# A fused attention, token-mixing and channel-mixing kernel: second tile's loads behind the first tile's heads, global-key terms on GpSimd, and three changes of order

## The reference, cut to what matters

```python
B, H, S, D = 2, 8, 768, 64                                # d_model = 512
scores = q @ k^T / 8 - slope_h * dist(is_global, is_local); masked by keep
a = exp(scores - max) / (sum + 1e-9);  x = a @ v          # [2, 768, 512]

h  = relu(x^T @ w_tok1) @ w_tok2                          # over tokens, 768 -> 256 -> 768
u  = x + h^T
x2 = u + relu(u @ w_ch1) @ w_ch2                          # 512 -> 1536 -> 512

theta = x2 @ w_theta                                      # 512 x 512
z_r, z_i = x2 * cos(theta), x2 * sin(theta)
y  = w_tok_r @ z_r + w_tok_i @ z_i                        # 768 x 768, over tokens
u2 = x2 + y
out = u2 + relu(u2 @ w_ch)                                # 512 x 512
```

## Time and profile before

| what | value |
|---|---|
| median of 3 timed runs | 496.13 us (496.01 to 496.19) |
| profiled execution | 497.82 us, of which span 496.0 us and 1.8 us around it |
| TensorE busy | 487.6 us (98% of the span) |
| VectorE, ScalarE, GpSimd busy | 325.8, 192.3, 267.7 us |
| mean granted TensorE clock | 0.996 |
| chain that ended last | TensorE 87%, VectorE 11%, the rest 2% |

### The profile page before, as it was taken

One profiled execution on the slowest core, in us unless ns is written; L12 is line 12 of the kernel. 1 busy time (PEld: TensorE's weight loads), 2 busy tenths in 40 slices (PEclk: granted clock), 3 DMA queues, 4 the chain that ended last, 5 costly groups with the idle time before them and its releaser, 6 DMA issues.

```text
span 496.0 us, 8394 instructions
## 1 busy us (share of the span) xinstructions
PE 487.6 (98%) x2917; PEld 445.6 (90%) x2917; DVE 325.8 (66%) x797; ACT 192.3 (39%) x413; POOL 267.7 (54%) x315
## 2 busy tenths in 40 slices
PE   7999999999999999999999999999989999999997
PEld 5999999899999999889999998888878899888897
DVE  7998999569535433399625436798887665655552
ACT  6999898555112121146112214344232321321230
POOL 3575566599798983739798882554930310000040
PEclk9999999999999999999999999999989999999999
DMA  7897675522132232104242242133102211000002
GB/s 239 326 304 242 239 219 147 157 85 84 58 95 85 83 110 85 44 0 128 64 129 85 72 134 72 65 110 125 42 2 60 67 66 64 0 1 0 2 32 96
DMA packets 27083, 49.81 MB, mean 100 GB/s; under 512 B 3360, under 2 KB 17696, under 8 KB 27040
## 3 DMA queue, kind: packets, MB, share of 16 engines
q1 hardware_dynamic: 27040, 49.26, 31.6%
HBM read 39.81 MB, written 3.15 MB: 87 GB/s over the span
## 4 chain that ended last, share of the span: by engine, by line
PE 87%; DVE 11%; issue 1%; ACT 1%; DMA 1%; DVEq 0%
PE bank L323 63%; PE bank L1800 7%; PE bank L1506 5%; PE bank L1536 4%; PE bank L1539 4%; PE bank L1520 2%; PE bank L1518 2%; DVE act_raw L1224 2%; DVE zc L1240 1%; DVE zs L1258 1%; DVE act_raw L1218 1%; DVE za L1234 1%; DVE tile L1202 1%; DVE zb L1253 1%; DMA counts<-both_counts 1%
## 5 line engine op out<-in xcount | busy, mean ns | idle before, releaser
L323 PE MATMUL bank<-wsplit 128*128 128x256 f32 (+2 forms) x816 | 148.8, 338 | 0.0
L323 PEld LDWEIGHTS bank<-wsplit 128*128 128x128 f32 x816 | 134.1, 188 | 13.3
L710 POOL TENSOR_TENSOR wsplit<-wraw,wsplit 128x512 fp32r<-128x512 f32 (+1 forms) x77 | 102.1, 1327 | 41.4 <-ACT wsplit L883 25.5
L323 PE MATMUL bank<-wsplit,zs 128*128 128x512 f32 (+1 forms) x576 | 105.0, 342 | 2.1 <-DVE zs L1258 2.1
L323 PEld LDWEIGHTS bank<-wsplit,zs 128*128 128x128 f32 x576 | 90.9, 191 | 16.7 <-issue 2.5
L778 POOL TENSOR_TENSOR split<-act_raw,split 128x384 fp32r<-128x384 f32 x12 | 12.5, 1079 | 105.5 <-ACT split L1008 105.5
L652 POOL TENSOR_TENSOR wsplit<-qk_raw,wsplit 64x256 fp32r<-64x256 f32 x46 | 38.0, 827 | 33.1 <-DVE wsplit L1051 32.8
L323 PE MATMUL bank<-split,wsplit 128*128 128x384 f32 x276 | 53.8, 339 | 0.4 <-DVE zb L1235 0.3
L704 POOL CAST wsplit<-wraw 128x512 fp32r<-128x512 f32 (+1 forms) x59 | 36.1, 612 | 26.9 <-PE bank L323 17.5
L323 PEld LDWEIGHTS bank<-split,wsplit 128*128 128x128 f32 x276 | 47.3, 188 | 1.1 <-DVE zb L1235 0.5
L1371 DVE SCALAR_TENSOR_TENSOR wsplit<-bank,wsplit 128x384 fp32r<-128x384 f32 x30 | 16.7, 558 | 38.1 <-ACT wsplit L961 26.9
(11 more groups left out here) (126 smaller groups left out, 749.9 us busy)
## 6 DMA issues: line engine op xcount, KB each, us to landing
wraw<-weights SPq DMA_DIRECT2D x28, 512.0 KB, 3.4
qk_raw<-qk SPq DMA_DIRECT2D x23, 528.0 KB, 4.5
wraw<-weights SPq DMA_DIRECT2D x8, 768.0 KB, 4.1
vt<-v SPq DMA_DIRECT2D x10, 520.0 KB, 4.6
xT<-turned SPq DMA_DIRECT2D x64, 48.0 KB, 2.0
out<-act_raw SPq DMA_DIRECT2D x16, 192.0 KB, 1.9
xT<-turned_early SPq DMA_DIRECT2D x16, 96.0 KB, 2.7
xT<-wraw SPq DMA_DIRECT2D x32, 48.0 KB, 2.0
```

Of the source, the lines that this page charges most:

```text
L323: mm = pe.matmul(dst, lhs(a), rhs(c), start=first and i == 0, stop=last and i == 2, skip_group_check=True)
L710: ins = pool.tensor_tensor(dst[:, cols], src[:, cols], hi[:, cols].bitcast(F32), ALU.subtract)
```

## The change

- SyncE waits for heads 4 to 7 of the first tile before it issues the second tile's transfers (and all that stands behind them).
- GpSimd instead of VectorE makes the global keys' terms and the first tile's bias of them, seven instructions instead of six, ahead of its first `queries_lo`. VectorE's wait for `slopes_ready` is gone; it waits for `gbias_ready` before it builds the other tiles' part.
- `WARM` goes from 13 to 11, `CHAN_FROM` from 3 to 5.
- VectorE makes `z_to_lo(g, 0)` before `tile_to_lo` and not behind it.
- For the last i of the last batch, TensorE makes three blocks and not two between `angles(0)` and the first product; one fewer stands at the end.

```diff
-WARM = 13
+WARM = 11
-CHAN_FROM = 3
+CHAN_FROM = 5
...
             load_queries_keys(0)
+            sp.wait_ge(qk_in[0][1], 16)
             for n in range(UNITS):
...
+            def find_global_terms():
+                ng, nl = cf[:, 0:1], cf[:, 2:3]
+                pool.tensor_scalar(c_gkey, c_gkey, ng, None, ALU.is_lt)
+                link(pool.tensor_scalar(c_gkeep, c_grel, nl, None, ALU.is_ge))
+                link(pool.tensor_tensor(c_gkeep, c_gkeep, c_gkey, ALU.mult))
+                pool.tensor_scalar(c_gdrop, c_gkeep, -MASKED, MASKED, ALU.mult, ALU.add)
+                link(pool.tensor_scalar(c_gdist, c_gkeep, nl, -1.0 / SCALE, ALU.mult, ALU.mult))
+
+            def first_global_bias():
+                heads = c_gheads[:, 0:H * G].rearrange("p (h g) -> p h g", h=H)
+                link(pool.tensor_tensor(heads, ..., ALU.mult))
+                pool.tensor_tensor(gbias[:, :, 0, :], heads, ..., ALU.add).then_inc(gbias_ready, 1)
...
             pool.wait_ge(slopes_ready, H)
+            pool.wait_ge(consts, 4)
+            pool.wait_ge(counts_ready, 1)
+            find_global_terms()
+            first_global_bias()
             for m in range(FIRST, PAIRS):
                 queries_lo(m)
...
             keys_lo(0, 0)
-            find_global_terms()
-            dve.wait_ge(slopes_ready, H)
-            build_global_bias(0, 1)
...
                 if m == PAIRS - 1:
+                    dve.wait_ge(gbias_ready, 1)
                     build_global_bias(1, 2)
...
                         multiply_x(g)
+                    if g >= 2 and not (b and s == 0):
+                        z_to_lo(g, 0)
                     if g >= 2 and g + 2 < B * T:
                         tile_to_lo(B * T + g + 2)
-                    if g >= 2 and not (b and s == 0):
-                        z_to_lo(g, 0)
...
                         angles(0)
-                        block(i - 1, *blocks[0])
-                        block(i - 1, *blocks[1])
+                        for at in range(3):
+                            block(i - 1, *blocks[at])
                         pe.wait_ge(th_taken, 1)
...
-                        block(i - 1, *blocks[2 if ahead else 0])
+                        block(i - 1, *blocks[3 if ahead else 0])
...
-                        block(i - 1, *blocks[3 if ahead else 1])
+                        block(i - 1, *blocks[4 if ahead else 1])
...
-                    block(i - 1, *blocks[4 if ahead else 2])
+                    block(i - 1, *blocks[5 if ahead else 2])
...
-                    block(i - 1, *blocks[5])
+                    block(i - 1, *blocks[6 if ahead else 5])
...
-                    block(i - 1, *blocks[6])
+                    if not ahead:
+                        block(i - 1, *blocks[6])
                     block(i - 1, *blocks[7])
```

More of the change, by code:

```diff
@@ L646, in _ @@
             link(pool.memset(half_pi[:, :], TWO_PI / 4))
+            def find_global_terms():
[7 more added lines that the diff above has]
+                heads = c_gheads[:, 0:H * G].rearrange("p (h g) -> p h g", h=H)
+                link(pool.tensor_tensor(heads, c_gdist[:, 0:G].unsqueeze(1).to_broadcast([P, H, G]),
+                                        slopes[:, :].unsqueeze(2).to_broadcast([P, H, G]), ALU.mult))
+                pool.tensor_tensor(gbias[:, :, 0, :], heads, c_gdrop[:, 0:G].unsqueeze(1).to_broadcast([P, H, G]),
+                                   ALU.add).then_inc(gbias_ready, 1)
             def queries_lo(m):
@@ L1074, in take_x @@
                                   ALU.mult).then_inc(x_done, 1)
[L1076 to L1081, removed]
             def build_global_bias(t, count):
```

## The result

| what | before | after |
|---|---|---|
| median of 6 runs each, one chip | 496.16 us (496.01 to 496.22) | 499.08 us (498.02 to 501.5) |
| ratio | | 1.0058, interval 1.0034 to 1.0081 |
| profiled execution | 497.82 us | 498.02 us |
| its span, its granted clock | 496.0 us, 0.996 | 496.2 us, 1.000 |

Slower by 2.9 us. The forecast was 495.2 us with a range to 497.6, and slower had a chance of 0.17.

What follows compares the result with a forecast made beforehand. TensorE bounds the kernel (busy 487.6 of 496.0 us), with one 2.1 us wait and 1.6 us of lower clock behind it. 497.82 + 1.4 - 2.3 = 496.9; from the median, 496.13 - 0.9 = 495.2 us; range 493.0 to 497.6.

Steps and rivals of the forecast that it cites:

- z_to_lo first: Near 360 us, tile 3: TensorE starts 1.4 us sooner and no clock fall follows; 3.0 us gained in total.
- What stays of the gain: Of the late part's 3.0 us, 2.3 us stay (bounds 1.7 and 3.0), since tile 5 is late next.
- The sum's base: The sum starts from the profiled execution, 497.82 us, clock fall included, and is then taken to the median, 496.13 us.
- rival 2: Timed runs hold the 2.1 us wait without the clock fall; only 0.7 us gained late; 496.8 us; chance 0.25.
- SyncE's wait: At the beginning, the second tile's half lands at 12.3 to 12.9 us; 1.4 us lost (0.7 gained to 2.0 lost).
- 1.3 MB in 3.2 us is the full rate of this queue: First transfers: second tile and values follow one another in the queue, and nothing of theirs holds up the first tile.
- Rival 1: First tile's heads land near 6.5 us, or the wait costs nothing; beginning gains 0.7 us; 493.1 us; chance 0.22.
- The global terms: At the beginning, GpSimd's seven instructions take 2.0 us, ending near 6.5; without the new wait, 0.5 to 0.7 us gained.
- The third block: Ahead of angles(1), a wait of 0.33 us becomes one of 0.5 us; 0.2 us lost (0.3 gained to 0.5 lost).
- rival 3: Gap in transfers idles TensorE at the first L1536 and lowers the clock; another 1.6 us lost; 497.4 us; chance 0.13.

Runs made afterwards that it cites:

- e8: Kernel before with CHAN_FROM 5 and z_to_lo ahead of tile_to_lo from tile 3 on, nothing else: 495.64 us, 0.9985.
- e10: Kernel before with SyncE's wait alone: 497.74 us, 1.0004.
- e14: Kernel before, old order, with two small ScalarE copies ahead of the last TOKRI rounding in tile 2: 497.61 us, a single execution.
- e2: Kernel before with only the change's beginning (SyncE's wait, global terms on GpSimd, WARM 11): 498.17 us, 1.0027.
- e9: Kernel before with the change's beginning but WARM left at 13: 496.52 us, 0.9988.
- e13: Kernel before, old order, with one small ScalarE copy ahead of the last TOKRI rounding in tile 2: 499.24 us, a single execution.
- e1: Kernel before with only the late part (z_to_lo ahead of tile_to_lo, CHAN_FROM 5, third block): 499.44 us, 1.0057.
- e11: Kernel before with z_to_lo ahead of tile_to_lo and one small ScalarE copy ahead of the last TOKRI rounding in tile 2: 498.95 us, 1.0041.
- e15: Kernel before with z_to_lo ahead of tile_to_lo and two small ScalarE copies ahead of the last TOKRI rounding in tile 2: 498.78 us, a single execution.
- e7: Kernel before with the third block alone: 496.64 us, 1.0004.
- e5: Kernel after, but with the old order, tile_to_lo ahead of z_to_lo, in tile 2 alone: 496.83 us, 1.0002.
- e6: Kernel after, with GpSimd's rests of the last TOKRI chunk held until tile 2's five additions are done: 497.65 us, 1.0006.
- e12: e8 with 4, 3, 3 filling matmuls instead of 2, 2, 2 in steps 0 to 2: 495.65 us, 0.9965 of before.

## Why the prediction was wrong, point by point

**z_to_lo first: wrong, and this is the main error.** I costed the swap where it was to help, in tile 3, and in tile 2 took it as "0.15 us in which VectorE now waits for ScalarE". In tile 2 five additions stand behind the swapped pair and beside GpSimd's rests, and the swap turned round which engine is held: 3.3 us more on VectorE, 3.0 us of waiting at `angles(4)`. I had used the stretching by GpSimd as a term in tile 3, so the mechanism was in hand; I did not look for the other places where the swapped code runs beside GpSimd. Before's own row, a GpSimd instruction of 2.98 us among ones of 1.35 and 1.63, shows that VectorE's pace there hung on who is held.

**What stays of the gain: right in kind.** Without tile 2's swap (e8) the wait at 360 us is 0.5 us, I said 0.5 to 0.7, and tile 5 is late next, by 0.6 us. At the level without a fall that gives 0.3 us by the lowest times (495.56 against 495.81) and 0.5 by the medians (495.64 against 496.18).

**The sum's base: rival 2 was right on this.** The timed runs beside the forecast, by their times, held the 2.1 us wait without the fall that followed it in the profile. So 0.7 us could be gained there, not 2.3. The fall is no sure companion of the wait: behind waits of 2.1 to 2.3 us at this place the traces of before, e10 and e14 have one of 3.41 us, those of e2, e9 and e13 none; after's and e1's 3.0 and 3.1 us had none behind them, e11's and e15's 3.1 and 3.2 had one. Rival 2's time, 496.8, missed all the same: it shared the other steps, the swap's above all, and had no falls in the runs after.

**SyncE's wait: the step that failed is "1.3 MB in 3.2 us is the full rate of this queue".** I read the landing at 8.5 us as set by the order in the queue alone. It was slowed by what stood behind: 6.1 to 6.5 us with the second tile queued, in eleven profiles, 4.8 to 5.0 without, in six. So the second tile, issued at 7.0, was ready at 10.67 and not at 12.3 or later; the loss is 0 and not 1.4 us. Rival 1 had it. The rule of the Trainium skill that the prediction weighed ("DMA: Bandwidth & Descriptors", Latency and other measured facts), a lighter load and a shorter latency, is borne out in direction, with 1.4 us for this transfer; whether it is the load of HBM or of the queue that counts, no run separates.

**The global terms: 2.0 us in the sum, 2.8 measured** (4.75 to 7.53), and begun 0.3 us later than I had it. I took seven instructions on 128x1 for seven on 128x24 and 128x64; `join_globals` moved from 7.53 to 7.56 us, and the gain of 0.5 to 0.7 us was 0.

**The third block: right.** 0.48 us of waiting before `angles(1)`, I said 0.5; start at 314.70, I said 314.55; 0.2 us lost by e7's medians, within their spread.

**The clock at the start: rival 3 had the kind, not the place.** I looked for idle time at the first L1536; there is none. The longest near the start, 1.2 us, lies between the first two steps, but the same wait stands in profiles with `WARM` = 13 and in profiles without a fall, so it is not shown to be the cause. What the counts show: of the kernels with `WARM` = 11 and the beginning's edits (after, e2, e5, e6) 34 of 42 runs had a fall, and 18 a clock of 0.993 or less; of before on the experiments' chips 52 of 96 and 12. With `WARM` back at 13 and the rest of the beginning kept (e9) it was 5 of 12 and none. That speaks for the shorter warming as what brings the longer falls, but e9 and e2 ran on two chips, and how often a fall comes differs from chip to chip for the same kernel; what starts one stays open.

## What to carry to other kernels

An order of instructions swapped inside a loop is to be costed in every pass of the loop, above all in those where VectorE and GpSimd both read SBUF: an instruction there that lasts twice its usual time on one engine shows that the other could be the one to wait. Compare times of like granted clock, and base a sum on a profiled execution only after seeing whether the timed runs are at its level. A reordering that pays in one pass can be limited to it, as in e8.

## What was not expected of the hardware

- Where VectorE's additions and GpSimd's rests meet, one engine is nearly stopped, and not both slowed a little: an addition of 0.42 us takes 1.51 us, or a rest of 1.35 us takes 2.98. Which one it is went with the order of two instructions of VectorE ahead of it.
- 528 KB land 4.8 to 5.0 us after their issue with nothing queued behind them, and 6.1 to 6.5 with 1.3 MB behind them.
- Stretches at half the clock lasted 3.41, 6.83 or 10.24 us. The first kind cost about 1.6 us behind the 2.1 us wait, the second, at the start, 2.5 (e8), the third 3.3 to 3.7 (e2). The same idle time of TensorE went with a fall in some executions and with none in others. A few more matmuls on ones in the first three steps (e12) went with no fall in 12 runs, beside 3 in 12 without them (e8, on another chip).
